# Products with 33 and 1 rows in a sparse-attention, channel-mix and Fourier kernel get 128 rows, the last key tile is turned as 64 columns

## The reference, cut to what matters

```python
# attention: 4 batches, 8 heads, 576 queries and keys, head size 64
scores = scale * np.matmul(q, k.transpose(0, 1, 3, 2))
thresh = np.max(scores, axis=-1, keepdims=True) - tau
scores = np.where(scores >= thresh, scores, -1000000000.0)
attn = softmax(scores)                      # with 1e-9 added to the row sum
x = np.matmul(attn, v)                      # heads side by side: (4, 576, 512)
# channel mix: each token and the one before it
k = np.maximum((mu_k * x + (1 - mu_k) * x_prev) @ w_k, 0.0)
r = sigmoid((mu_r * x + (1 - mu_r) * x_prev) @ w_r)
x = r * (k * k @ w_v)
# Fourier mixing, layer norm, dense layers of 512 -> 2048 -> 512
u = x + np.real(np.fft.fft(np.fft.fft(x, axis=1), axis=2))
un = (u - mean) / np.sqrt(var + 1e-6)
out = u + np.maximum(un @ w_ch1, 0.0) @ w_ch2
```

## Time and profile before

| | |
|---|---|
| median of three executions | 1114.38 us (1113.59 to 1114.43) |
| profiled execution: its own time | 1115.46 us |
| profiled execution: span from first to last instruction | 1113.7 us |
| PE busy | 1078.5 us, 97% of the span |
| DVE, ACT, POOL busy | 551.7, 512.7, 420.0 us (50%, 46%, 38%) |
| mean granted clock of TensorE | 0.988 of full speed |

### The profile page before, as it was taken

The page is one execution under the profiler, slowest core; times in us unless marked ns, Lnnn a source line. Parts: engine busy times, 40 slices in busy tenths (PEclk is TensorE's granted clock), DMA queues, the critical chain, the costliest instruction groups (busy, mean ns, idle before and its releaser), DMA issues.

```text
span 1113.7 us, 18462 instructions
## 1 busy us (share of the span) xinstructions
PE 1078.5 (97%) x7088; PEld 1012.4 (91%) x7088; DVE 551.7 (50%) x1081; ACT 512.7 (46%) x1250; POOL 420.0 (38%) x360
## 2 busy tenths in 40 slices
PE   7999999999999999999998999999999999999998
PEld 6899999998899998899997998888888888888998
DVE  7988764466565566565563655334114123223211
ACT  5979876646675646775644643221111111111110
POOL 5887653533663433763413445351111111111000
PEclk9989999999899999999999899999999999999999
DMA  8635111042121032121022207300200200200000
GB/s 237 176 98 170 37 43 34 24 140 53 65 56 35 23 104 89 66 57 34 2 71 77 105 1 287 122 1 1 69 1 1 69 1 1 68 1 1 35 1 33
DMA packets 37251, 69.30 MB, mean 62 GB/s; under 512 B 4134, under 2 KB 18604, under 8 KB 36140
## 3 DMA queue, kind: packets, MB, share of 16 engines
q1 hardware_dynamic: 36860, 67.80, 19.5%
q10 hardware_dynamic: 304, 0.33, 0.1%
HBM read 55.84 MB, written 12.28 MB: 61 GB/s over the span
## 4 chain that ended last, share of the span: by engine, by line
PE 82%; POOL 6%; DVE 4%; issue 3%; ACT 3%; DMA 0%; SPq 0%; DVEq 0%; POOLq 0%; ACTq 0%
PE PB L731 20%; PE PB L733 19%; PE PB L732 19%; PE PB L788 10%; PE PB L758 6%; PE PB L771 6%; POOL mix_l L630 1%; DVE probs L1284 1%; POOL x2T L662 1%; DVE neg_s L1270 1%; POOL q_hl L579 1%; POOL x2T L663 1%; POOL k_lo L571 1%; ACT exps L1019 1%; POOL fold_l L651 1%
## 5 line engine op out<-in xcount | busy, mean ns | idle before, releaser
L1228 ACT ACTIVATE h_hi<-PB 128x464 fp32r<-128x464 f32 (+1 forms) x80 | 44.5, 556 | 335.6 <-PE PB L733 335.6
L1461 DVE SCALAR_TENSOR_TENSOR h_lo<-PB,h_hi 128x464 fp32r<-128x464 f32 (+1 forms) x80 | 51.0, 638 | 264.0 <-ACT h_hi L1228 264.0
L788 PE MATMUL PB<-v_sb,probsT 128*128 128x64 f32 (+1 forms) x1440 | 180.2, 273 | 0.0
L788 PEld LDWEIGHTS PB<-v_sb,probsT 128*128 128x128 f32 x1440 | 175.1, 195 | 0.0
L1028 ACT ACTIVATE probsT<-PB 128x384 f32<-128x384 f32 (+1 forms) x288 | 109.5, 433 | 84.5 <-PE PB L771 83.5
L1284 DVE SCALAR_TENSOR_TENSOR probs<-neg_s,thresh,exps 128x576 f32<-128x576 f32 x144 | 145.7, 1012 | 0.3 <-PE PB L771 0.3
L1270 DVE TENSOR_SCALAR_CACHE_REDUCE neg_s<-PB,taus 128x576 f32<-128x576 f32 x144 | 117.1, 814 | 42.4 <-PE PB L758 38.1
L731 PE MATMUL PB<-un_h,w1h 128*128 128x464 f32 (+1 forms) x320 | 121.7, 380 | 0.0
L733 PE MATMUL PB<-un_h,w1l 128*128 128x464 f32 (+1 forms) x320 | 118.9, 371 | 0.0
L732 PE MATMUL PB<-h_lo,w2h 128*128 128x464 f32 (+1 forms) x320 | 118.8, 371 | 0.0
L731 PE MATMUL PB<-h_hi,w2h 128*128 128x464 f32 (+1 forms) x320 | 118.8, 371 | 0.0
(11 more groups left out here) (154 smaller groups left out, 2398.6 us busy)
## 6 DMA issues: line engine op xcount, KB each, us to landing
q_raw<-qT_dram SPq DMA_DIRECT2D x62, 160.0 KB, 3.2
k_raw<-kT_dram SPq DMA_DIRECT2D x64, 144.0 KB, 3.2
w_raw<-w_dram SPq DMA_DIRECT2D x8, 1024.0 KB, 9.3
cs<-cs_scr SPq DMA_DIRECT2D x4, 1740.0 KB, 8.0
u_scr<-x2T SPq DMA_DIRECT2D x4, 1152.0 KB, 5.2
cd<-cd_scr SPq DMA_DIRECT2D x4, 1032.0 KB
v_sb<-v_dram SPq DMA_DIRECT2D x16, 256.0 KB, 2.9
u_in<-u_scr SPq DMA_DIRECT2D x4, 928.0 KB, 6.1
```

The lines of the kernel that those rows point to most:

```text
L788: last = nc.tensor.matmul(bank(6 + p)[:, i * DH:i * DH + width], probsT[:, n % 2, kt * P128:(kt + 1) * P128], v_sb[:, kt, pair % 2, p * DH ...
L1461: nc.vector.scalar_tensor_tensor(h_lo[:, ft % 3, 0:w], bank(4 + ft % 3)[:, 0:w], 0.0, h_hi[:, ft % 3, 0:w].bitcast(F32), ALU.max, ALU.subt ...
```

## The change

- U: the third tile of `y_h` gets memory of its own (`y_h2`, in the place of `mean512` and of the 64 spare columns of `probs`), and so does that of `y_l` (`y_l2`). POOL zeroes both at the start; ACT and DVE write the first 33 rows as before. PE contracts over 128 rows in all three tiles. `y_l2` shares its bytes with the gate of batch 3, so POOL zeroes it once more there, when the gate has been read.
- Y: `odd`, `mid_v`, `mid_h` and `mid_l` are filled in all 128 rows. `odd` is zero in all but row 0. PE contracts over 128 rows in L841 and L842. The three DMAs of `odd` move 128 rows of 1032 B.
- Attention: the fifth transpose of a tile takes 64 columns of `probs` and writes 64 partitions; the other 64 partitions of that place in bank 5 are zeroed once by DVE, in place of the two fills of `probs`. PE's first fifth transpose waits for it (`tail_zero`).
- `mean512` moves into the memory of the last part, and POOL fills it in batch 3, when the memory is free (after the first load of u).

```diff
-        mean512 = m.put("mean512", [P128, P128], F32)
+        y_h2 = m.put("y_h2", [P128, 2 * KC], F32R)
-        probs = m.put("probs", [P128, 2, KT * P128], F32)
+        probs = m.put("probs", [P128, 2, S], F32)
...
-                    sp.dma_start(odd[0:1, :], odd_scr).then_inc(cd_in, 16)
+                    sp.dma_start(odd[:, :], odd_scr).then_inc(cd_in, 16)
...
             def _(pool):
-                nc.gpsimd.memset(mean512[:, :], 1.0 / D)
                 nc.gpsimd.memset(rowsum[:, :], 1.0).then_inc(pool_ready, 1)
+                nc.gpsimd.memset(y_h[ST - 1][:, :].bitcast(F32), 0.0)
+                nc.gpsimd.memset(y_l[ST - 1][:, :].bitcast(F32), 0.0).then_inc(y_padded, 1)
...
                             yield MIX_AT[7] + 1
+                            pool.wait_ge(u_loaded[0], 16)
+                            nc.gpsimd.memset(mean512[:, :], 1.0 / D)
                             sum_u(0, 0, 1)
...
-                            nc.gpsimd.tensor_tensor(mid_l[0:1, 0:NYQ], mid_v[0:1, 0:NYQ], mid_h[0:1, 0:NYQ].bitcast(F32), ALU.subtract).then_inc(foldl_ready, 1)
+                            nc.gpsimd.tensor_tensor(mid_l[:, 0:NYQ], mid_v[:, 0:NYQ], mid_h[:, 0:NYQ].bitcast(F32), ALU.subtract).then_inc(foldl_ready, 1)
                             pool.wait_ge(foldl_ready, d * 5 + 3)
+                            if alone(d):
+                                pool.wait_ge(x2_ready, d * 8 + 8)
+                                nc.gpsimd.memset(y_l[ST - 1][:, :].bitcast(F32), 0.0).then_inc(y_padded, 1)
...
-                            last = nc.tensor.transpose(bank(4 + unit % 2)[:, (kt - k0) * P128:(kt - k0 + 1) * P128],
-                                                       probs[:, n % 2, kt * P128:(kt + 1) * P128], ident[:, :])
+                            keys = min(P128, S - kt * P128)
+                            if n == 0 and keys < P128:
+                                pe.wait_ge(tail_zero, 1)
+                            last = nc.tensor.transpose(bank(4 + unit % 2)[0:keys, (kt - k0) * P128:(kt - k0 + 1) * P128],
+                                                       probs[:, n % 2, kt * P128:kt * P128 + keys], ident[:, :])
...
-                        nc.tensor.matmul(o, mid_h[0:1, ss], odd[0:1, :].bitcast(F32R), start=False, stop=False)
-                        nc.tensor.matmul(o, mid_l[0:1, ss], odd[0:1, :].bitcast(F32R), start=False, stop=False)
+                        nc.tensor.matmul(o, mid_h[:, ss], odd[:, :].bitcast(F32R), start=False, stop=False)
+                        nc.tensor.matmul(o, mid_l[:, ss], odd[:, :].bitcast(F32R), start=False, stop=False)
...
-                            rows = SROWS[st]
                             if g < 2:
                                 pe.wait_ge(yl_ready, d * 6 + 2 * st + g + 1)
-                            last = three(ring(d, "u", 0, g)[:, 0:FS], y_h[0:rows, st, c0:c0 + P128], y_l[st][0:rows, c0:c0 + P128],
-                                         cs[0:rows, 0, st, cols].bitcast(F32R), cs[0:rows, 1, st, cols].bitcast(F32R), st == 0, st == ST - 1)
+                            last = three(ring(d, "u", 0, g)[:, 0:FS], y_h[st][:, c0:c0 + P128], y_l[st][:, c0:c0 + P128],
+                                         cs[:, 0, st, cols].bitcast(F32R), cs[:, 1, st, cols].bitcast(F32R), st == 0, st == ST - 1)
...
+                        if st == ST - 1:
+                            act.wait_ge(y_padded, 1)
...
+                nc.vector.memset(bank(5)[64:128, P128:2 * P128], 0.0).then_inc(tail_zero, 1)
...
-                    if n < 2:
-                        nc.vector.memset(probs[:, n, S:KT * P128], 0.0).then_inc(tail_zero, 1)
...
+                        if alone(d) and st == ST - 1:
+                            dve.wait_ge(y_padded, 2)
```

More of the change, by code:

```diff
@@ L269, in build @@
         at_end = m.at
-        y_l1 = [m.put(f"y_l{st}", [P128, 2 * KC], F32R) for st in (1, 2)]
+        y_l2 = m.put("y_l2", [P128, 2 * KC], F32R)
         gate_alone = Place(at_end).put("gate_alone", [P128, DT, HALF], F32)
@@ L289, in build @@
         cs = r.put("cs", [P128, 2, ST, 2 * FS], F32)
-        y_h = r.put("y_h", [P128, ST, 2 * KC], F32R)
-        y_l = [r.put("y_l0", [P128, 2 * KC], F32R)] + y_l1
+        y_h = [r.put(f"y_h{st}", [P128, 2 * KC], F32R) for st in (0, 1)] + [y_h2]
+        y_l = [r.put(f"y_l{st}", [P128, 2 * KC], F32R) for st in (0, 1)] + [y_l2]
         assert r.at <= at_end
@@ L344, in build @@
         w2_parts = [put_w2(r, r, 0)]
+        mean512 = r.put("mean512", [P128, P128], F32)
         assert r.at <= at_xT
@@ L359, in build @@
         put_un(r, low)
-        assert r.at <= at_ksq and low.at <= m.at
+        assert r.at <= at_ksq and low.at <= top
         w2h, w2_raw, w2l = [[part[i] for part in w2_parts] for i in range(3)]
@@ L402, in build @@
         dft_ready, qcp_ready, ab_ready, row_copied = [sem(n) for n in ("dft_r", "qcp_r", "ab_r", "row_copied")]
-        u_part, u_stored = sem("u_part"), sem("u_stored")
+        u_part, u_stored, y_padded = sem("u_part"), sem("u_stored"), sem("y_padded")
         w1_in = [sem(f"w1_in{i}") for i in range(4)]
@@ L520, in _ @@
                     if n == 15:
-                        sp.dma_start(odd_raw[0:1, :], dft_odd).then_inc(odd_raw_in, 16)
+                        sp.dma_start(odd_raw[:, :], dft_odd).then_inc(odd_raw_in, 16)
                     if 15 <= n < 15 + KFT:
@@ L530, in _ @@
                         sp.dma_start(cs_scr[:, 1], cs_lo[:, :, :].bitcast(F32)).then_inc(tables_stored, 16)
-                        sp.dma_start(odd_scr, odd_r[0:1, :].bitcast(F32)).then_inc(tables_stored, 16)
+                        sp.dma_start(odd_scr, odd_r[:, :].bitcast(F32)).then_inc(tables_stored, 16)
                     run_beside(beside, n)
@@ L1070, in weight_hi @@
                         act.wait_ge(odd_raw_in, 16)
-                        nc.scalar.activation(odd_r[0:1, :], odd_raw[0:1, :], ACT.Copy).then_inc(odd_rounded, 1)
+                        nc.scalar.activation(odd_r[:, :], odd_raw[:, :], ACT.Copy).then_inc(odd_rounded, 1)
                     t -= ST + 6
@@ L1157, in dense @@
                             act.wait_ge(fold_ready, d * 5 + 3)
-                            nc.scalar.activation(mid_h[0:1, 0:NYQ], mid_v[0:1, 0:NYQ], ACT.Copy).then_inc(foldh_ready, 1)
+                            nc.scalar.activation(mid_h[:, 0:NYQ], mid_v[:, 0:NYQ], ACT.Copy).then_inc(foldh_ready, 1)
                     for g in range(2 * ST):
@@ L1163, in dense @@
                         act.wait_ge(y_ready, d * 6 + g + 1)
-                        nc.scalar.activation(y_h[0:rows, st, kind * KC:(kind + 1) * KC], ring(d, "y", 0, g)[0:rows, 0:KC], ACT.Copy).then_inc(yh_ready, 1)
+                        if st == ST - 1:
+                            act.wait_ge(y_padded, 1)
+                        nc.scalar.activation(y_h[st][0:rows, kind * KC:(kind + 1) * KC], ring(d, "y", 0, g)[0:rows, 0:KC], ACT.Copy).then_inc(yh_ready, 1)
                     for pr in range(2):
@@ L1203, in _ @@
                 act.wait_ge(pool_ready, 1)
-                nc.scalar.activation(exps[:, 0, 0:1], mean512[:, 0:1], ACT.Exp)
+                nc.scalar.activation(exps[:, 0, 0:1], rowsum[:, 0:1], ACT.Exp)
                 act.wait_ge(qk_in[0], 64)
@@ L1412, in dense @@
                         dve.wait_ge(yh_ready, d * 6 + g + 1)
+                        if alone(d) and st == ST - 1:
+                            dve.wait_ge(y_padded, 2)
                         nc.vector.tensor_tensor(y_l[st][0:rows, kind * KC:(kind + 1) * KC], ring(d, "y", 0, g)[0:rows, 0:KC],
-                                                y_h[0:rows, st, kind * KC:(kind + 1) * KC].bitcast(F32), ALU.subtract).then_inc(yl_ready, 1)
+                                                y_h[st][0:rows, kind * KC:(kind + 1) * KC].bitcast(F32), ALU.subtract).then_inc(yl_ready, 1)
                     for pr in range(2):
@@ L1437, in middle @@
                 def middle(d):
-                    nc.vector.tensor_copy(mid_v[0:1, ends], x2T[0:1, 3, ends])
-                    nc.vector.tensor_tensor(mid_v[0:1, near], x2T[0:1, 3, near], x2T[0:1, 3, far], ALU.add).then_inc(fold_ready, 1)
+                    nc.vector.tensor_copy(mid_v[:, ends], x2T[:, 3, ends])
+                    nc.vector.tensor_tensor(mid_v[:, near], x2T[:, 3, near], x2T[:, 3, far], ALU.add).then_inc(fold_ready, 1)
                 beside = [[Beside(mixing(d)), Beside(dense(d))] for d in range(B)]
@@ L1521 @@
     dft_d[:, KC:KC + D // 2] = np.sin(ang[:, :D // 2])
-    dft_odd = np.zeros((1, KC))
+    dft_odd = np.zeros((P128, KC))
     dft_odd[0, 1:D // 2:2] = -2.0
@@ L1548 @@
     cd_scr = nc.dram_tensor("cd_scr", (P128, 2, 2, 2 * KC), F32, kind="Internal").ap()
-    odd_scr = nc.dram_tensor("odd_scr", (1, KC), F32, kind="Internal").ap()
+    odd_scr = nc.dram_tensor("odd_scr", (P128, KC), F32, kind="Internal").ap()
     cs_scr = nc.dram_tensor("cs_scr", (P128, 2, ST, 2 * FS), F32, kind="Internal").ap()
```

## The result

The changed kernel takes 1103.74 us in the median of six runs (1101.89 to 1108.19), the kernel before 1114.93 us beside it; the ratio is 0.9906, with a 95% interval of 0.9885 to 0.9927. The forecast was 1107.3 us in a range of 1102.8 to 1112.0. The direction and the range hold; the gain looks 3.6 to 4.1 us larger than the forecast 7.1 us (against the forecast time, and against the kernel before beside it), and that difference is what the experiments are about.

What follows compares the result with a forecast made beforehand. PE was taken to bound the kernel: busy 97% of the span, 82% of the chain. Batches 0 to 3 gave 1.975 + 1.975 + 1.195 + 1.95 = 7.1 us, so 1114.38 - 7.1 = 1107.3 us, range 1102.8 to 1112 us.

Steps and rivals of the forecast that it cites:

- the terms of the sum: PE time saved by removed changes of rows: 1.975 us in each of batches 0 and 1, 1.195 in 2, 1.95 in 3.
- The lost changes: Changes of rows whose removal gains nothing because PE waits anyway, among them seven of U in batch 2, six of Y in batch 3.
- The step that the chain did not show: Batches 0 and 1, U: three changes before `q_cp` count, since `q_cp` delays `mix_h`, which POOL awaits; 0.195 us each.
- The fifth transpose: Attention, 144 times: the stream of 128 elements sets its pace, so 64 instead of 128 columns change nothing; taken as 0.
- the 0.055 us of the rival: Fifth transpose: loading weights sets part of its pace, so 128 columns cost up to 0.055 us a tile more, 7.9 us over 144.
- The way back from 64 to 128 columns: First product with v behind every fifth transpose, 144 times: 0 to 0.195 us each, 0 to 28 us; taken as 0.
- The clock takes part back: PE's longer wait for `mix_l` in batches 0 and 1 brings stretches at 1.2 GHz, 3.4 us each; one 15%, two 4%.
- the stalls stay: PE's stalls belong to something other than the number of rows, such as the wait before each group; 1114.4 us, 4%.
- the load of the weights: Fifth transpose: loading weights sets its pace, so 64 columns save 7.9 us more, giving 1099.4 us; 5%.
- the stall at 64 columns: Return from 64 to 128 columns stalls the first product with v, up to 0.195 us, 144 times, giving 1135 us; 6%.
- 39 of 64: Changes of rows on PE predicted to lie on the path, out of all in U and the single-row pairs; 7.1 of 11.8 us.
- the bound from a subtraction: POOL's fills: 516 columns cost at most what a subtraction of that size does, 1.48 us; `mean512` under the same bound.

Runs made afterwards that it cites:

- 16 fillers: Changed kernel, or kernel before, with 16 extra overwritten PE products (26 in batch 3) ahead of the first `mix_l` of batches 1 to 3: mean 1098.84, 1106.91 us.

## Why the prediction was right

The profiled runs of the changed kernel and of the kernel before with 16 fillers are the cleanest pair: between the rows below the clock falls only once, in the first: from 660 to 668 us it is 0.79, a loss of 1.7 us. That is between the fourth row and the fifth, 64.78 against 63.05 us, a stretch that I leave out, since the clock accounts for the 1.73 us. PE in order of time, changed with fillers: first products of Y in batches 0, 1 and 2, first product of k in batch 3, first of Y and of U there, and the first of the dense layers.

```profile
246.79 0.37 PE L741 MATMUL PB<-cd,fold_h 128*128 128x258 f32 x1
411.54 0.37 PE L741 MATMUL PB<-cd,fold_h 128*128 128x258 f32 x1
575.78 0.36 PE L741 MATMUL PB<-cd,fold_h 128*128 128x258 f32 x1
609.27 0.30 PE L741 MATMUL PB<-mix_h,wkh 128*128 128x288 f32 x1
674.05 0.28 PE L741 MATMUL PB<-cd,fold_h 128*128 128x258 f32 x1
681.46 0.37 PE L741 MATMUL PB<-cs,y_h 128*128 128x290 f32 x1 [0.61 <-DVE y_l L1431]
687.54 0.38 PE L741 MATMUL PB<-un_h,w1h 128*128 128x464 f32 x1
```

The same seven of the kernel before with fillers:

```profile
245.73 0.37 PE L731 MATMUL PB<-cd,fold_h 128*128 128x258 f32 x1
412.61 0.37 PE L731 MATMUL PB<-cd,fold_h 128*128 128x258 f32 x1
578.96 0.36 PE L731 MATMUL PB<-cd,fold_h 128*128 128x258 f32 x1
613.61 0.30 PE L731 MATMUL PB<-mix_h,wkh 128*128 128x288 f32 x1
676.66 0.28 PE L731 MATMUL PB<-cd,fold_h 128*128 128x258 f32 x1
683.91 0.37 PE L731 MATMUL PB<-cs,y_h 128*128 128x290 f32 x1 [0.38 <-DVE y_l L1416]
691.83 0.48 PE L731 MATMUL PB<-un_h,w1h 128*128 128x464 f32 x1
```

The distances, before against after, answer to the terms of the sum one by one:

| stretch | before | after | gain | forecast |
|---|---|---|---|---|
| batch 0, Y to Y | 166.88 | 164.75 | 2.13 | 1.975 |
| batch 1, Y to Y | 166.35 | 164.24 | 2.11 | 1.975 |
| batch 2, Y to batch 3's k | 34.65 | 33.49 | 1.16 | 1.195 |
| batch 3, Y | 7.25 | 7.41 | -0.16 | 0 |
| batch 3, U to the dense layers | 7.92 | 6.08 | 1.84 | 1.95 |
| sum | | | 7.08 | 7.1 |

The stretches outside the table matter too. Ahead of the first row the changed kernel is 1.06 us later, though neither run loses clock there. It is no fixed cost of the change: the same row stands at 245.93 us in the first profiled run of the changed kernel, and at 245.72 and 245.37 us in those with U at 33 rows and `mid` at one row. Where the 1.06 us come from is not shown. With them, the 1.73 us, and 0.11 us gained behind the last row, the two whole spans, 1102.8 and 1098.4 us, differ by 4.4 us only; a single pair of runs does not show the 7.1 us without such a table.

*What is on the path.* The lost changes were lost: in batch 3 the wait in front of U grows from 0.38 to 0.61 us, and Y gains nothing; in batch 2 seven changes of U go into the wait for POOL. The step that the chain did not show, three changes on PE ahead of `q_cp` counted though the chain stood on POOL, held as well: with those three (0.6 us) left out, batches 0 and 1 would have been at 1.4, not 2.1 us.

*The fifth transpose* costs nothing either way by its rows; with 128 columns put back the kernel is 0.4 to 0.7 us slower in span times clock, with a standard error of 0.4, so at most some 0.01 us a tile, and not the 0.055 us of the rival. The way back from 64 to 128 columns, for which before had no row, is free: 0.54 us for the five in both.

*The rivals.* "The clock takes part back" named the right place: the wait grew, and the fall came in batch 1 too. But the profiled run of the changed kernel lost two other falls, and over many runs the clock is the same, 0.9896 before and 0.9903 after. That the stalls stay, the load of the weights and the stall at 64 columns are refuted by the rows.

*The size.* The term that the first six runs seemed to show too small was none of the sum's. At nearly full clock the gain is 7.1 us. Without fillers it is 8.6 us with a standard error of 0.7; 0.8 us of it is the clock's 0.0007 over 1112 us. The remaining 0.7 us is no more than its error and stays open; that stretches at 1.2 GHz fall into the changed kernel's longer waits more often, where they cost less, would fit, but was not measured.

## What to carry to other kernels

Price a removed stall from the distance of two neighbours on the chain, then decide batch by batch whether the engine is the one waited for at that place: 39 of 64 counted here, and the 7.1 us came out at 7.1 with a standard error of 0.3. Look one step behind a wait that the chain puts down to another engine, since an earlier result can shorten it. And before a gain of less than 1% is explained, compare the granted clock of the runs: kernels kept near full clock, compared at the same clock, resolved what 13 and 54 plain runs left open.

## What the runs showed of the hardware

A wait of PE had a second price here, beside its length. In the changed kernel waits of 2.8 to 3.1 us in three places stood next to stretches at 1.2 GHz; I estimate that all such stretches made up 21 us of a run (0.0097 x 1103 us x 2, since such a stretch counts half). With needless products ahead of the waits 5 us are left, and the kernel is 5.7 us faster by the means, though PE has 75 products more to do; with 16 fillers and a wait of 1.0 us left in two of the places the clock was still 0.998. The length of one wait does not decide it, though: a wait of 2.7 us went with 0.94 in one batch and with 1.00 in the next. Nor are these three places the only ones. In the profiled run with 16 fillers and `mid` at one row the clock was 0.991, and the falls stood in the first batch, where no fillers are: 0.72 from 32 to 44 us, 0.79 from 48 to 56 and 0.63 from 62 to 76, each beside a wait of PE of 1.3 to 1.7 us. Fillers in three places raise the clock of most runs, not of all.

POOL's fills were far cheaper than the bound from a subtraction: 516 columns in 0.53 us, against the 1.48 us taken from the earlier trace rows, and the 128 columns of `mean512` in 0.20 us.
